# First channel projection of three of four mixers as seven block products, with their preparation moved into the mixer before

## The reference

```python
# attention: q, k, v are (2, 8, 768, 64); window 128 and 4 sink keys
keep = is_sink | in_window
x = softmax(where(keep, q @ k.T / 8, -1e9)) @ v        # x: (2, 768, 512)
# layer 1: U (768, 32), V (32, 768), w_ch1 (512, 2048), w_ch2 (2048, 512)
u = x + (x.T @ U @ V).T
x = u + maximum(u @ w_ch1, 0) @ w_ch2
# layer 2: w_tok1 (768, 256), w_tok2 (256, 768), w_ch1 (512, 1536), w_ch2 (1536, 512)
u = x + (maximum(x.T @ w_tok1, 0) @ w_tok2).T
out = u + maximum(u @ w_ch1, 0) @ w_ch2
```

## Time and profile before

| what | value |
|---|---|
| median of 3 runs | 673.14 us (672.04 to 675.73) |
| span of the profiled execution, first to last instruction | 671.3 us |
| own time of the profiled execution | not given apart from its span; the median of the runs is 1.8 us above the span |
| PE busy | 651.1 us, 97% of the span |
| DVE, ACT, POOL busy | 31%, 44%, 56% |
| granted TensorE clock, mean | 0.997 |
| HBM traffic | 112 GB/s over the span |
| attention of batch 0 | 0 to 87 us |
| mixer (1,0) with attention of batch 1 | 87 to 278 us |
| mixers (2,0), (1,1), (2,1) | 278 to 400, 400 to 545.5, 545.5 to 668 us |

### The profile page before, as it was taken

The page is one execution under the profiler, slowest core; times in us unless marked ns, Lnnn a source line. Parts: engine busy times, 40 slices in busy tenths (PEclk is TensorE's granted clock), DMA queues, the critical chain, the costliest instruction groups (busy, mean ns, idle before and its releaser), DMA issues.

```text
span 671.3 us, 10346 instructions
## 1 busy us (share of the span) xinstructions
PE 651.1 (97%) x3652; PEld 587.5 (88%) x3652; DVE 204.9 (31%) x526; ACT 296.1 (44%) x693; POOL 372.9 (56%) x393
## 2 busy tenths in 40 slices
PE   6889999999999999999999999999999999999998
PEld 5878798989999899899999988999999989999996
DVE  7776552333353331231121123111311134012112
ACT  4656565445464444373333324333433347233331
POOL 8544466646555545545665653666666654566562
PEclk9999899999999999999999999999999999999999
DMA  8334254352323333424445442544444442444541
GB/s 182 90 80 111 48 142 125 97 133 79 103 83 91 95 83 106 122 77 116 126 126 172 125 126 59 160 126 127 116 124 128 123 123 80 117 128 126 163 125 63
DMA packets 119955, 76.00 MB, mean 113 GB/s; under 512 B 43968, under 2 KB 103872, under 8 KB 119904
## 3 DMA queue, kind: packets, MB, share of 16 engines
q1 hardware_dynamic: 119904, 75.34, 40.4%
HBM read 71.91 MB, written 3.15 MB: 112 GB/s over the span
## 4 chain that ended last, share of the span: by engine, by line
PE 91%; DVE 4%; issue 2%; ACT 1%; POOL 1%; DMA 0%; DVEq 0%; ACTq 0%; POOLq 0%
PE bank L959 35%; PE bank L984 35%; PE bank L842 4%; PE bank L869 4%; PE bank L850 3%; PE bank L943 3%; PE bank L906 2%; PE bank L887 2%; PE bank L827 1%; PE bank L924 1%; PE bank L980 1%; DVE k_hi L711 1%; DVE masked L727 1%; DVE x_nat L754 1%; DVE sums_eps L749 1%
## 5 line engine op out<-in xcount | busy, mean ns | idle before, releaser
L575 POOL TENSOR_TENSOR w_lo<-w_raw,w_hi 128x512 fp32r<-128x512 f32 (+1 forms) x238 | 301.8, 1286 | 202.1 <-ACT w_hi L596 201.7
L672 DVE SCALAR_TENSOR_TENSOR hid_lo<-bank,hid_hi 128x384 fp32r<-128x384 f32 x112 | 62.4, 558 | 351.9 <-ACT hid_hi L584 351.9
L584 ACT ACTIVATE hid_hi<-bank 128x384 fp32r<-128x384 f32 x112 | 55.0, 491 | 246.5 <-PE bank L959 246.4
L959 PE MATMUL bank<-uT_hi,w_hi 128*128 128x384 f32 x448 | 153.1, 342 | 0.0
L959 PE MATMUL bank<-uT_hi,w_lo 128*128 128x384 f32 x448 | 151.1, 337 | 0.0
L959 PE MATMUL bank<-uT_lo,w_hi 128*128 128x384 f32 x448 | 150.6, 336 | 0.0
L596 ACT ACTIVATE w_hi<-w_raw 128x512 fp32r<-128x512 f32 (+1 forms) x238 | 138.1, 618 | 1.2 <-PE bank L906 1.2
L984 PE MATMUL bank<-w_hi,hid_hi 128*128 128x512 f32 x336 | 134.1, 399 | 0.0
L984 PE MATMUL bank<-w_hi,hid_lo 128*128 128x512 f32 x336 | 132.7, 395 | 0.0
L984 PE MATMUL bank<-w_lo,hid_hi 128*128 128x512 f32 x336 | 132.3, 394 | 0.0
L959 PEld LDWEIGHTS bank<-uT_hi,w_hi 128*128 128x128 f32 x448 | 84.3, 188 | 3.7 <-DVE uT_lo L675 0.2
(11 more groups left out here) (82 smaller groups left out, 628.5 us busy)
## 6 DMA issues: line engine op xcount, KB each, us to landing
w_raw<-in_moe_w_ch_dram SPq DMA_DIRECT2D x224, 256.0 KB, 2.8
q_nat<-in_q_dram SPq DMA_DIRECT2D x12, 256.0 KB, 3.0
k_nat<-in_k_dram SPq DMA_DIRECT2D x12, 256.0 KB, 3.6
v_nat<-in_v_dram SPq DMA_DIRECT2D x12, 256.0 KB, 3.2
out_dram<-o_stage SPq DMA_DIRECT2D x12, 256.0 KB, 3.3
w_raw<-in_moe_w_tok_dram SPq DMA_DIRECT2D x6, 256.0 KB, 2.9
w_raw<-in_moe_w_tok_dram SPq DMA_DIRECT2D x8, 192.0 KB, 2.3
U_sb<-in_moe_U_dram SPq DMA_DIRECT2D x3, 96.0 KB, 3.3
```

The costliest lines, as they stand in the source:

```text
L575: nc.gpsimd.tensor_tensor(w_lo[:, split % NW, 0:n], w_raw[:, split % NR, 0:n], w_hi[:, split % NW, 0:n].bitcast(f32), ALU.subtract) \
L584: nc.scalar.activation(dst, m_tile(key)[0:rows, 0:dst.shape[-1]], func).then_inc(hi_ready, 1)
L672: nc.vector.scalar_tensor_tensor(out=dst, in0=src, scalar=0.0, in1=hi.bitcast(f32), op0=ALU.max, op1=ALU.subtract).then_inc(m_drained, 1)
L959: last = mm(m_tile(use)[:, 0:HALF], w[:, slot, rows], u[:, kk, cols], start=(n == 0), stop=(n == 3 * KD - 1))
```

## The change

Mixer (1,0) stays as it is. In the other three, `mm1` for a pair of hidden blocks (256 columns, both halves of the tokens) becomes one product of 2 by 2 blocks: the weights are cut by channels and by hidden block (A11, A12, A21, A22, each 256 channels by 128), u transposed by channels and by token half (B11, B12, B21, B22, each 256 by 384). Seven block products replace eight. Each is 6 matmuls of 384 columns (two 128-channel tiles by three parts). The plan order is now (1,0), (1,1), (2,0), (2,1).

- **`s1`, `s2`** (per pair): four products, then three more, into four PSUM banks. ACT copies the first product out, DVE adds banks and copies to the four results: C11 and C21 (first token half, used by `mm2` at once), C12 and C22 (second token half, kept in `hid2`, 128 x 16 x 384).
- **`wsplit`, `wsum`, `wload`** (per pair): one DMA of 512 KB for both blocks; DVE builds four sums of weight blocks (128x256 each); ACT rounds and POOL subtracts for seven weight parts (128x512, 128x256, 128x1024). These weights are now loaded and split once, not once per token half.
- **`ysplit`**: the second token half of a block is split out of `hid2` (ACT, then DVE) just before its `mm2`. In that second half only `mm2` steps run on PE.
- **`bprep`** (once per mixer, in two parts): the seven parts of u. ACT rounds seven blocks of 128x768; POOL subtracts for three of them (B11, B21, B22); DVE builds four sums T1, T2, T4, T3 and subtracts for these (eight instructions of 128x768).
- **Places.** `down`, `up` and `bprep` of a mixer are put between the `mm2` steps of the second half of the mixer before it (steps f = 1 to 7). For (1,1) they stand between `mm1` and `mm2` steps in the second half of (1,0); to make room there, attention of batch 1 gives two units instead of one behind every third step.
- `mm2` steps, their matmuls and their weight chunks are unchanged in number.

```diff
+    def preparation(layer, b):
...
+            units = [split[0]] + [[("down", 2, b, c)] + split[c + 1] for c in range(NQ // 2)]
+        units.append([("up", layer, b, 0)])
+        units.append([("up", layer, b, 1), ("bprep", layer, b, 0)])
+        units.append([("bprep", layer, b, 1)])
+        return units
+    def seven(layer, b, between):
...
+        for g in range(last + 1):
+            at = pair_at[layer, b, g]
+            steps.append(("s1", layer, b, g))
+            if at + 1 < NPAIRS:
+                steps.append(("wsplit", at + 1))
+            if g:
+                steps.append(("mm2", layer, b, 0, 2 * g - 2))
+            steps.append(("s2", layer, b, g))
+            if at + 2 < NPAIRS:
+                steps.append(("wsum", at + 2))
...
+            if g:
+                steps.append(("mm2", layer, b, 0, 2 * g - 1))
...
+        for f in range(FCH[layer]):
+            steps.append(("mm2", layer, b, 1, f))
+            if f + 2 < FCH[layer]:
+                steps.append(("ysplit", layer, b, f + 2))
+            if f and between:
+                steps += between.pop(0)
...
-    waiting = attention(1)
-    for s in mixer(1, 0, down=False):
+    waiting = attention(1) + preparation(1, 1)
+    waiting[-2] += [("wload", 0), ("wload", 1), ("wsum", 0), ("wsplit", 0)]
+    waiting[-1] += [("wsum", 1), ("wload", 2)]
+    n = 0
+    for s in mixer(1, 0):
...
+            n += 1
             plan += waiting.pop(0)
+            if n % 3 == 0 and len(waiting) > len(preparation(1, 1)):
+                plan += waiting.pop(0)
     assert not waiting
-    plan += mixer(2, 0) + mixer(1, 1) + mixer(2, 1)
+    plan += seven(1, 1, preparation(2, 0)) + seven(2, 0, preparation(2, 1)) + seven(2, 1, [])
...
+        FIRST = ((A11, B11, 0), (S2, T2, 1), (S3, T3, 2), (S1, T1, 3))
+        SECOND = ((A12, B21, 0), (A22, T4, 2), (S4, B22, 3))
...
+                elif s[0] == "bprep" and s[3] == 1:
...
+                    nc.vector.tensor_tensor(t_sum["T1"], u_quarter(0, 1), u_quarter(0, 0), ALU.subtract) \
+                      .then_inc(t_summed, 1)
+                    dve.wait_ge(t_summed, summed + 1)
+                    nc.vector.tensor_tensor(t_sum["T2"], u_quarter(2, 1), t_sum["T1"], ALU.subtract) \
+                      .then_inc(t_summed, 1)
+                    dve.wait_ge(b_high, high + 1)
+                    nc.vector.tensor_tensor(b_lo[:, T1], t_sum["T1"], b_hi[:, T1].bitcast(f32), ALU.subtract) \
+                      .then_inc(t_low, 1)
...
+            def product(s, at, a, b_part, z, first):
...
+                for k in range(2):
+                    for w, u in ((a_hi, b_hi), (a_hi, b_lo), (a_lo, b_hi)):
+                        last = mm(bank[:, 0:HALF], w[:, at % 2, a, k, :], u[:, b_part, k, :],
+                                  start=(first and n == 0), stop=(n == 5), skip_group_check=True)
+                        n += 1
+                last.then_inc(p_ready, 1)
...
+                elif s[0] == "s2":
+                    at = pair_at[s[1:]]
+                    for (a, b_part, z), read_out in zip(SECOND, (p1_copied, u3_ready, c22_ready)):
+                        pe.wait_ge(read_out, at + 1)
+                        product(s, at, a, b_part, z, False)
```

More of the change, by code:

```diff
@@ L106, in attention, with mixer @@
         return units
-    def mixer(layer, b, down=True):
-        steps = [("down", layer, b, i) for i in range(NQ if layer == 1 else NQ // 2)] if down else []
-        steps += [("up", layer, b, half) for half in range(2)]
+    def mixer(layer, b):
+        steps = [("up", layer, b, half) for half in range(2)]
         hidden = [(layer, b, half, f) for half in range(2) for f in range(FCH[layer])]
@@ L117, in mixer, with pairs_until @@
         return steps
-    plan = [s for unit in attention(0) for s in unit] + [("down", 1, 0, NQ - 1)]
-    waiting = attention(1)
-    for s in mixer(1, 0, down=False):
+    SEVEN = [(1, 1), (2, 0), (2, 1)]
+    pair_at = {}
+    for layer, b in SEVEN:
+        for g in range(FCH[layer] // 2):
+            pair_at[layer, b, g] = len(pair_at)
+    NPAIRS = len(pair_at)
+    pairs = list(pair_at)
+    def pairs_until(layer, b):
+        return pair_at[layer, b, FCH[layer] // 2 - 1] + 1
+    def preparation(layer, b):
+        if layer == 1:
+            units = [[("down", 1, b, 2 * c), ("down", 1, b, 2 * c + 1)] for c in range(NQ // 2)]
+        else:
+            split = [[("xsplit", b, 2 * c), ("xsplit", b, 2 * c + 1)] for c in range(NQ // 2)] + [[]]
+            units = [split[0]] + [[("down", 2, b, c)] + split[c + 1] for c in range(NQ // 2)]
[3 more added lines that the diff above has]
+        return units
@@ new lines, in seven @@
+    def seven(layer, b, between):
+        steps = []
+        last = FCH[layer] // 2 - 1
+        for g in range(last + 1):
[8 more added lines that the diff above has]
+                steps.append(("wsum", at + 2))
+            if at + 3 < NPAIRS:
+                steps.append(("wload", at + 3))
+            if g:
+                steps.append(("mm2", layer, b, 0, 2 * g - 1))
+        steps += [("ysplit", layer, b, 0), ("ysplit", layer, b, 1)]
+        steps += [("mm2", layer, b, 0, 2 * last), ("mm2", layer, b, 0, 2 * last + 1)]
+        for f in range(FCH[layer]):
[4 more added lines that the diff above has]
+                steps += between.pop(0)
+        assert not between
+        return steps
@@ L186, in attention_then_two_mixers @@
                 open_bank((s, d), up_bank(s, d))
-                close_bank((s, d), True)
+                close_bank((s, d), s[1:3] == (1, 0))
         elif s[0] == "mm1":
@@ L190, in attention_then_two_mixers @@
             close_bank((s, 0), True)
+        elif s[0] == "s1" and s[3] == 0:
+            for n in range(4):
+                open_bank(("z", s[1], s[2], n), Z_BANKS[s[1:3]][n])
         elif s[0] == "mm2":
@@ L251, in attention_then_two_mixers @@
+        A11, A12, A22, S1, S2, S3, S4 = range(7)
+        B11, B21, B22, T1, T2, T4, T3 = range(7)
+        FIRST = ((A11, B11, 0), (S2, T2, 1), (S3, T3, 2), (S1, T1, 3))
+        SECOND = ((A12, B21, 0), (A22, T4, 2), (S4, B22, 3))
         banks = [ctx.enter_context(nc.psum_tensor(f"bank{i}", [P, DM], f32)) for i in range(8)]
@@ L501, in _ @@
                         loaded += 1
-                if s[0] == "mm1" and s[4] == 2:
+                if s[0] == "wload":
+                    load_pair(s[1])
+                if s[0] == "mm2" and s[3:] == (1, 4) or s[0] == "s2" and s[3] == 1:
                     while stores:
@@ L934, in _ @@
                         rows = slice(d * P, (d + 1) * P)
+                        if d >= early:
+                            transposes(d)
                         if layer == 1:
```

371 lines of the change are left out of this document (306 added, 65 removed).

## The result

| what | before | changed |
|---|---|---|
| median of the runs | 672.59 us (671.8 to 675.73) | 704.29 us (701.4 to 706.25) |
| ratio | 1 | 1.0465 (95% interval 1.0431 to 1.0498) |
| span of the profiled execution | 671.3 us | 701.4 us |
| granted TensorE clock, mean | 0.997 | 0.976 |

What follows compares the result with a forecast made beforehand. PE was taken as the bound, busy 651.1 of 671.3 us. The sum 671.3 - 21.0 - 5.5 + 4.4 + 17.0 + 24.0 + 5.1 gave a 695.3 us span, 697 us on the median, range 674 to 706.

Steps and rivals of the forecast that it cites:

- What PE saves: Mixers' products: 960 matmuls become 840, saving 21.0 us; with the head waits 26.5 us.
- three head waits: Heads of three mixers: waits of 2.06, 2.06 and 1.36 us go, 5.5 us gained.
- Attention pressed together: Mixer (1,0), ten steps with two heads in a row: costs 4.4 us, bounds 0 and 8.
- the second head's wait for the score bank: Attention pairs in (1,0): scores wait about 0.15 us for the bank DVE reads, at each of ten pairs.
- The waits for probs_T: Attention pairs in (1,0): product with the values waits 0.53 us where ACT copies, 0.05 where DVE does, five each.
- The pair loop: Products per pair: PE has 11.5 us, POOL 7.0, DVE 5.6, ACT under 5; costed at nothing.
- The preparation of u: `bprep` ahead of the products: PE waits 17.0 us in (1,0), 12.0 us each in (1,1) and (2,0).
- One queue for both engines: In `bprep`, DVE's two-SBUF instructions and POOL's do not overlap, less 0.1 us at each hand-over.
- the rival of side by side: DVE and POOL overlap in `bprep`: 666 to 670 us with clock held (0.11), 671 to 675.5 with clock fallen (0.09).
- The clock: Behind each of three new gaps the granted clock falls, losing 1.7 us each, 5.1 us; bounds 0 and twice that.
- The range: Whole kernel's median: 8 in 10 range 674 to 706 us; the forecast's own range 685 to 706.

Runs made afterwards that it cites:

- the filler: Changed kernel plus 40 unread matmuls of 512 columns ahead of block 10 in (1,1) and (2,0): 700.70 us, ratio 1.0433.
- spreading alone: Changed kernel with one head a step, sums and low parts of T1 to T4 spread over five steps, preparation earlier, nothing from PSUM: 680.0 us, ratio 1.0117.
- the kernel with sums from PSUM and one head a step: Changed kernel with B11, B21, B22 and T1 to T3 formed from PSUM banks, and one head behind each step of (1,0): 676.87 us, ratio 1.0055.
- the kernel of 660.56 us: The kernel with sums from PSUM and one head a step, with low parts spread over four steps, (1,1)'s preparation and first weight sums moved: ratio 0.9829.

## Why the prediction was right or wrong

- **What PE saves: right for the products, wrong for the heads.** 840 products' matmuls at 0.174 us save 20.9 us. The 5.5 us for three head waits were never PE's: the sum took the ACT and DVE pieces of the chain for idle time of PE, which was transposing x and stood for about 0.1 us at each head. Some 1.1 us are measured there.
- **Attention pressed together: the step that failed most.** It was priced at 4.4 us with bounds of 0 to 8; alone it costs 14.4. The sum took the second head's wait for the score bank as 0.15 us, 1.5 us for ten pairs, from a head with an idle DVE. Measured are 0.54 to 1.66 us at the six pairs behind an `mm1`, 5.6 us together, because DVE's masking stands behind the step's hid_lo, and that behind ACT. The waits for probs_T were about right (3.6 us for 2.9). The remainder, a wait of 1.7 us and 3 to 4 us in the spacing of the matmuls, has no term in the sum, and its cause stays open. The bound was wrong as well, since it was drawn from the same head. I had written down what the head's own chain needs and left out what is queued ahead of it on DVE and ACT.
- **The pair loop: right**, at nothing: 11.48 us a pair.
- **The preparation of u: right in kind, high in size.** The gaps are 10.55 us each for a forecast of 12.0; in (1,0) the waits are 10.9 us for 17.0, and `mm2` 9 starts 2.4 us earlier than worked out, since part of the time until then goes into matmuls at the half clock. One queue for both engines, against the rival of side by side: the timeline shows the turns, and less work of POOL's shortened DVE's gap.
- **The clock: right in kind, low in size.** 2.2 us at each of the two large gaps for a forecast of 1.7; the filler gave back 3.6 us for two.
- **The range** held the time, in part by luck of signs: attention and the heads came out 14.1 us worse than their terms, the gaps with the clock 5.9 us better (40.2 for 46.1) and all other steps 2.1 us better. The attention term is the one that I had looked up in a single head.

What is not settled: why a pair of heads behind an `mm2` costs over 1 us, and mixer (1,0)'s gap, whose waits were not taken apart further. I did not try to give attention a second score bank, since all eight banks are in use there.

## What to carry to other kernels

A piece of the chain of waits that ACT or DVE sets is not yet a wait of PE: look in PE's timeline for what it does meanwhile, before the piece is counted as time to be gained. Before two units that were apart are put side by side, write down what each engine's queue holds ahead of the first one's last instruction, and not only the unit's own chain; a wait that a long PE step hides costs its full length once that step is gone. Where DVE instructions with two SBUF inputs and POOL's stand in one stretch, add their times as one queue and set it against PE's time there; if it is nearly full, spreading alone cuts the gap into pieces (9.3 us for 10.55 in mixer (1,1) here), and taking inputs from PSUM makes room. When a change saves work on the bound engine and still loses, look first at whether its preparation can be made cheaper: here 32 us of loss turned into 12 us of gain.

## What the runs showed of the hardware

- DVE and POOL do not keep each other out for long: with both queues full they take turns instruction by instruction, so that the shorter suffers most. A weight sum of 0.42 us takes 1.50 beside chunks of 1.29, and L1016 in the changed kernel averages 2738 ns where L1031, the same form, has 957. The page "SBUF — State Buffer" of the Trainium skill, in "Who interferes with whom", says that a DVE instruction with two SBUF inputs contends with a GpSimd one that reads SBUF, over a port pair that is an exclusive lock (that the loser fully blocks, as the prediction has it, stands there for DVE's two-port modes). The trace agrees for one instruction (1.98 us for a chunk of 1.29 that began 0.85 us before DVE was done), and shows in addition that the next turn is then the loser's.
- A DVE instruction with an input in PSUM is not slowed by POOL: a b_lo from the bank takes 0.55 us, as without POOL, beside a running a_lo of POOL of 1.29 (283.66 and 283.77, in the kernel with sums from PSUM and one head a step).
- Behind a gap of 10.55 us PE works at 1.2 GHz for another 4.4 us, and with the gap filled by unread matmuls not at all. In the kernel of 660.56 us the granted clock is 1.00 from 431 to 439 us, around the two waits of 1.2 us, and 0.50 from 279 to 285 us, behind the one of 3.70 us in `up`.
